# Evicting both banks of turned probabilities with one instruction per engine in place of two, in a one-core attention and MLP kernel

## The reference

```
mask   = q_assign[:, :, :, None] == k_assign[:, :, None, :]
scores = scale * np.matmul(q, k.transpose(0, 1, 3, 2))
scores = np.where(mask, scores, -1000000000.0)
attn   = np.exp(scores - max) / (sum + 1e-09)
out    = np.matmul(attn, v)
```

## Time and profile before

| | us |
|---|---|
| median of 3 runs | 789.22 |
| lowest and highest | 788.41, 789.59 |
| time of the profiled execution | 788.7 |
| its span, first to last instruction | 786.9 |
| attention, first to last turn (L1069) | 24.0 to 300.0 |

### The profile page before, as it was taken

One profiled execution on the slowest core, in us unless ns is written; L12 is line 12 of the kernel. 1 busy time (PEld: TensorE's weight loads), 2 busy tenths in 40 slices (PEclk: granted clock), 3 DMA queues, 4 the chain that ended last, 5 costly groups with the idle time before them and its releaser, 6 DMA issues.

```text
span 786.9 us, 11657 instructions
## 1 busy us (share of the span) xinstructions
PE 738.2 (94%) x4073; PEld 651.2 (83%) x4073; DVE 418.3 (53%) x787; ACT 328.9 (42%) x678; POOL 251.2 (32%) x244
## 2 busy tenths in 40 slices
PE   2899999999999997998999999999999988899998
PEld 1788888888888887997888888888888878898886
DVE  4688788887888888576421141113111158885320
ACT  2677777778777775221111111111101036443311
POOL 5555455556655504002840000000014034641000
PEclk9999999999999999999999999999999999999999
DMA  3223322223343102001310000001013042000011
GB/s 102 70 68 74 92 68 63 63 66 103 109 134 99 43 1 74 35 1 55 108 52 1 0 1 1 1 0 55 1 33 127 1 133 55 28 14 28 27 41 53
DMA packets 20450, 40.93 MB, mean 52 GB/s; under 512 B 2753, under 2 KB 7105, under 8 KB 19905
## 3 DMA queue, kind: packets, MB, share of 16 engines
q1 hardware_dynamic: 17968, 31.62, 14.3%
q0 software_dynamic: 2448, 8.87, 3.4%
HBM read 31.04 MB, written 3.15 MB: 43 GB/s over the span
## 4 chain that ended last, share of the span: by engine, by line
PE 73%; DVE 11%; ACT 8%; issue 6%; POOL 1%; DMA 0%; DVEq 0%; ACTq 0%; SPq 0%; POOLq 0%
PE ps L1162 23%; PE ps L1241 17%; PE ps L1320 9%; PE ps L1306 5%; PE ps L1083 4%; PE ps L1069 4%; PE ps L1057 3%; PE ps L1030 3%; ACT prob L512 2%; PE ps L1058 2%; ACT k L502 2%; DVE row_min L706 2%; ACT pt_h L524 1%; PE ps L1093 1%; ACT q L501 1%
## 5 line engine op out<-in xcount | busy, mean ns | idle before, releaser
L924 DVE SCALAR_TENSOR_TENSOR hid_l<-ps,hid_h 128x512 fp32r<-128x512 f32 x48 | 33.2, 691 | 203.0 <-ACT hid_h L612 203.0
L713 DVE TENSOR_TENSOR pt_l<-ps,pt_h 128x384 fp32r<-128x384 f32 x192 | 102.5, 551 | 47.5 <-ACT pt_h L524 47.2
L612 ACT ACTIVATE hid_h<-ps 128x512 fp32r<-128x512 f32 x48 | 28.7, 598 | 227.0 <-PE ps L1162 227.0
L524 ACT ACTIVATE pt_h<-ps 128x384 fp32r<-128x384 f32 x192 | 84.0, 489 | 48.8 <-PE ps L1069 48.2
L706 DVE TENSOR_REDUCE row_min<-ps 128x1 f32<-128x768 f32 x96 | 90.3, 940 | 6.5 <-PE ps L1058 6.5
L512 ACT ACTIVATE prob<-ps,row_min 128x768 f32<-128x768 f32 x96 | 86.8, 905 | 1.9 <-DVE row_min L706 1.5
L1069 PE MATMUL ps<-cst,prob 128*128 128x128 f32 x576 | 83.4, 282 | 2.9 <-ACT prob L512 2.8
L1057 PE MATMUL ps<-k,q 80*128 80x384 f32 x192 | 74.9, 390 | 3.4 <-ACT k L502 1.5
L1162 PE MATMUL ps<-un_h,w_h 128*128 128x512 f32 x192 | 75.7, 394 | 1.4 <-DVE un_l L918 1.4
L1241 PE MATMUL ps<-w_h,hid_h 128*128 128x512 f32 x192 | 76.0, 396 | 0.0
L1162 PE MATMUL ps<-un_l,w_h 128*128 128x512 f32 x192 | 75.6, 394 | 0.0
(11 more groups left out here) (138 smaller groups left out, 1570.8 us busy)
## 6 DMA issues: line engine op xcount, KB each, us to landing
stage<-in_moe_w_ch SPq DMA_DIRECT2D x16, 256.0 KB, 3.3
w_raw<-in_moe_w_ch SPq DMA_DIRECT2D x16, 256.0 KB, 2.6
raw_qk<-in_q SPq DMA_DIRECT2D x16, 192.0 KB, 3.2
raw_qk<-in_k SPq DMA_DIRECT2D x16, 192.0 KB, 3.4
raw_v<-in_v SPq DMA_DIRECT2D x16, 192.0 KB, 2.5
q<-q SPq DMA_DIRECT2D x16, 192.0 KB, 2.6
k<-k SPq DMA_DIRECT2D x16, 192.0 KB, 2.6
out<-out_s SPq DMA_DIRECT2D x12, 256.0 KB, 2.0
```

What stands on the lines that cost most here:

```text
L524: nc.scalar.activation(pt_h[a][:, R * hf:R * hf + R, (t % R) * P:(t % R + 1) * P], ps[:, 4 + hf, 0:HALF].rearrange("p (j c) -> p j c", j=R ...
L713: nc.vector.tensor_tensor(pt_l[a][part], ps[:, 4 + hf, 0:HALF].rearrange("p (j c) -> p j c", j=R), as_f32(pt_h[a][part]), ALU.subtract).th ...
```

## The change

Both halves are evicted together. TensorE waits once for `low_ready` before the six transposes, and counts `turn_ready` once behind the sixth. `store_high` is one Copy of 768 columns from banks 4 and 5, and `store_low` one subtraction of 768 columns. The counts of the semaphores halve. VectorE's instructions of the mask chain, which stood between two halves of `store_low`, now stand behind the whole; `denominator` is moved in the same way.

```diff
             def store_high(n, t):
-                for hf in range(2):
-                    act.wait_ge(turn_ready, 2 * g + hf + 1)
-                    if t % R == 0 and hf == 0 and not (isinstance(n, int) and n == 0):
-                        act.wait_ge(o_ready, AHEAD + 2 * n + a - 1)
-                    nc.scalar.activation(
-                        pt_h[a][:, R * hf:R * hf + R, (t % R) * P:(t % R + 1) * P],
-                        ps[:, 4 + hf, 0:HALF].rearrange("p (j c) -> p j c", j=R),
-                        ACT.Copy).then_inc(high_ready, 1)
+                act.wait_ge(turn_ready, g + 1)
+                if t % R == 0 and not (isinstance(n, int) and n == 0):
+                    act.wait_ge(o_ready, AHEAD + 2 * n + a - 1)
+                nc.scalar.activation(
+                    pt_h[a][:, :, (t % R) * P:(t % R + 1) * P].rearrange("p (h j) c -> p h j c", h=2),
+                    ps[:, 4:6, 0:HALF].rearrange("p h (j c) -> p h j c", j=R),
+                    ACT.Copy).then_inc(high_ready, 1)
...
-            def store_low(n, t, hf):
+            def store_low(n, t):
                 g, a = 6 * n + t, t // R
-                dve.wait_ge(high_ready, 2 * g + hf + 1)
...
+                dve.wait_ge(high_ready, g + 1)
+                part = (slice(None), slice(None), slice((t % R) * P, (t % R + 1) * P))
+                nc.vector.tensor_tensor(pt_l[a][part].rearrange("p (h j) c -> p h j c", h=2),
+                                        ps[:, 4:6, 0:HALF].rearrange("p h (j c) -> p h j c", j=R),
+                                        as_f32(pt_h[a][part]).rearrange("p (h j) c -> p h j c", h=2),
+                                        ALU.subtract).then_inc(low_ready, 1)
...
-                store_low(m, 1, 0)
+                store_low(m, 1)
                 if prep2:
                     add_dots(n + 2)
-                store_low(m, 1, 1)
                 if prep2:
                     largest_dot(n + 2)
                 minimum(m, 1 - s, 3)
                 if prep2:
                     hits(n + 2)
-                store_low(m, 2, 0)
+                store_low(m, 2)
                 if prep2:
                     weigh_hits(n + 2)
-                store_low(m, 2, 1)
                 if prep2:
                     first_hit(n + 2)
                     masks(n + 2)
...
                 pe.wait_ge(exp_ready, g + 1)
+                if not (isinstance(g, int) and g == 0):
+                    pe.wait_ge(low_ready, g)
                 for hf in range(2):
-                    if not (isinstance(g, int) and g == 0):
-                        pe.wait_ge(low_ready, 2 * g - 1 + hf)
                     for j in range(R):
                         last = nc.tensor.transpose(ps[:, 4 + hf, j * P:(j + 1) * P],
                                                    prob[t % 2][:, R * hf + j, :], ident)
-                    last.then_inc(turn_ready, 1)
+                last.then_inc(turn_ready, 1)
```

More of the change, by code:

```diff
@@ L509, in exponent @@
                 if not (isinstance(g, int) and g < 2):
-                    act.wait_ge(turn_ready, 2 * g - 2)
+                    act.wait_ge(turn_ready, g - 1)
                 col = 6 * s + t
@@ L707, in minimum @@
                                         axis=AX.XY, op=ALU.min).then_inc(min_ready, 1)
-            def store_low(n, t, hf):
+            def store_low(n, t):
                 g, a = 6 * n + t, t // R
-                dve.wait_ge(high_ready, 2 * g + hf + 1)
-                part = (slice(None), slice(R * hf, R * hf + R), slice((t % R) * P, (t % R + 1) * P))
-                nc.vector.tensor_tensor(pt_l[a][part], ps[:, 4 + hf, 0:HALF].rearrange("p (j c) -> p j c", j=R),
-                                        as_f32(pt_h[a][part]), ALU.subtract).then_inc(low_ready, 1)
+                dve.wait_ge(high_ready, g + 1)
[4 more added lines that the diff above has]
+                                        ALU.subtract).then_inc(low_ready, 1)
             def add_dots(n):
@@ L775, in step @@
             def step(n, s, t, more=True):
-                store_low(n, t, 0)
-                store_low(n, t, 1)
+                store_low(n, t)
                 if t < 4:
@@ L794, in head @@
                 step(n, s, 4, more=prep1)
-                store_low(n, 5, 0)
+                store_low(n, 5)
                 denominator(n, s, 0)
-                store_low(n, 5, 1)
                 invert(n, 0)
@@ L807, in head @@
                 minimum(m, 1 - s, 1)
-                store_low(m, 0, 0)
+                store_low(m, 0)
                 denominator(n, s, 1)
-                store_low(m, 0, 1)
                 invert(n, 1)
@@ L1070, in turn @@
                                                    prob[t % 2][:, R * hf + j, :], ident)
-                    last.then_inc(turn_ready, 1)
+                last.then_inc(turn_ready, 1)
             def values(n, s, a, part):
                 if part == 0:
-                    pe.wait_ge(low_ready, 12 * n + 6 * a + 6)
+                    pe.wait_ge(low_ready, 6 * n + 3 * a + 3)
                     pe.wait_ge(v_split, n + 1)
```

## The result

The changed kernel takes 820.65 us (median of 4, 819.88 to 824.62) against 788.82 before: a ratio of 1.0414, with a 95% interval of 1.0392 to 1.0437. The forecast was 803.0 with a range of 798.5 to 808.0. The sign was right and the size was not: of the 32 us lost, the sum had 14.

A forecast was written before the change was run, and what follows sets the result against it. TensorE's work bounds most of a head, a VectorE and ScalarE chain bounds m3; heads 10.2, end 2.0, behind the last turn 0.6 and opening 1.0 make 13.8 us more, forecast 803.0, range 798.5 to 808.0.

The forecast's parts named there:

- heads, loop and mask chain: In the 14 heads with a mask, the mask comes 0.73 us later in each: 10.2 us.
- opening steps: Three first steps that wait in the same way, at the loop's 0.37 us each: about 1.0 us.
- end, to the last turn: Six last steps without a mask, 2.76 us each, 16.56 in place of 14.54: 2.0 us more.
- behind the last turn: VectorE's last low part starts later, with the next stage's subtractions behind it: 0.6 us.
- Low path: From turn to turn through Copy and subtraction of 768 columns: 2.71 to 2.76 us, becoming the loop over TensorE's 2.44.
- the replay: One head stepped through from the turn of m1, Copy starting at 0.85, mask turn at 6.81 us, before 6.08.
- the mask chain: VectorE's work from m1 to the mask turn in m3: the mask comes 0.73 us later.
- its cover: In t5 the loop of 2.76 us fits under the step's 3.01: no cost.
- Faster: Rival: fewer VectorE starts shorten the mask chain of m1 and m2; 2.0 us less, 787.2; chance 0.03.
- Hidden: Rival: late turns of m1 and m2 only eat into TensorE's waits; only the ends cost 3.6, 792.8; chance 0.06.
- Slow forms: Rival: the two-bank Copy and subtraction run at their upper bounds; 811 us; chance 0.08.
- Clock: Rival: idling TensorE falls to half clock in one step a head; 34 us more, 837; chance 0.01.

The follow-up runs named there:

- e2: Changed kernel with GpSimd's `split_v` of a head waiting for that head's mask (`mask_ready`); 807.26 us.
- e10: Kernel before the change with only GpSimd's `split_v` waiting for the mask; 787.46 us, ratio 0.9982.
- e1: Changed kernel without VectorE's `denominator`: the 1e-9 is left out and `invert` reads `row_sum` itself; 815.84 us.
- e4: Control: kernel before the change, with `denominator` left out and `split_v` waiting for the mask; 786.83 us, ratio 0.9977.
- e9: Kernel before plus GpSimd's wait for the mask; TensorE counts `turn_ready` once, so ScalarE's first Copy waits for six transposes; all instructions in halves; 805.67 us.
- e5: Kernel before plus GpSimd's wait for the mask; `turn_ready` counted once, one Copy of 768 columns, subtraction and TensorE's turn wait still in halves; 804.64 us.
- e7: Kernel before plus GpSimd's wait for the mask; only the waits merged (ScalarE for six transposes, turn for both low halves), four instructions in halves; 806.11 us.
- e11: Kernel before plus GpSimd's wait for the mask, VectorE's mask chain one place forward, one k mask eviction moved from ScalarE to VectorE; 781.82 us, ratio 0.9905.

## Why the prediction was wrong

Its sum, term by term, against the traces (14 heads with a mask):

| term | predicted | measured | from |
|---|---|---|---|
| heads, loop and mask chain | 10.2 | 13.7 | 14 x (18.38 - 17.40), e2 |
| `masks` beside GpSimd | 0 | 9.0 | 14 x (4.50 - 3.86), m3 |
| `denominator` beside GpSimd | 0 | 6.2 | 14 x (3.27 - 2.83), m1 |
| opening steps | 1.0 | 2.4 | 16.6 - 14.2 |
| end, to the last turn | 2.0 | 2.4 | 20.0 - 17.6 |
| behind the last turn | 0.6 | 0 | 487.5 in both |
| start of the first turn | 0 | -1.2 | 22.84 against 24.05 |
| sum | 13.8 | 32.5 | spans: 32.3 |

The first two rows set e2, in which GpSimd waits, against the kernel before, in which it does not. Against e10, which has the same wait, the heads' loop and chain are 14 x (18.38 - 17.29) = 15.3, and `masks` is so much less (7.4, since the kernel before already lost 1.5).

**The step that failed** is the sentence on the other engines: "GpSimd, SyncE and their DMAs get no instruction and no wait more; their waits are on steps that come later, and so start later with them". That is true and beside the point. It looked at what GpSimd waits for, and put what VectorE meets beside it at nothing. GpSimd's work on v starts when the values of m2 are through, so it moves with TensorE: 2.80 behind the turn of m2 before, 2.79 now. `masks` stands 2.99 behind that turn before and 3.35 now. Before, `masks` ran from 121.91 to 122.50: it lost 0.17 to GpSimd's first instruction for v (121.72 to 122.23) and was nearly through when the subtraction for v started at 122.32. Now it starts with that subtraction, and its second instruction waits for the end of it.

The other half of the failed step is "VectorE's `denominator` and `invert` stand behind a whole low part now; they are read by `store_x`, which waits for `fold_o`, so no cost". Behind the whole low part `denominator` starts 2.63 or 2.71 us behind the turn of m0, where it was 1.58 or 1.66. GpSimd's first instruction on k stays about where it was behind that turn, 2.31 to 3.36 now and 2.58 to 3.28 before. So a margin of 0.96 to 1.70 us fell to between -0.40 and 0.65, which is why 8 heads pay and 6 do not. The two together are 15.2 of the 18.7 us that the sum was short. e2 takes `masks` out and e1 `denominator`, and e4 shows that the kernel before has only the 0.17 a head of `masks`. The largest of the other misses are m0, 14 x 0.19 = 2.7, and the opening, 1.4.

The Trainium skill, SBUF — State Buffer, section SBUF: two separate sides, states the mechanism: VectorE and GpSimd share a pair of ports as an exclusive lock, taken for a whole instruction by a VectorE instruction in a two-port mode or with two inputs in SBUF (this one only against a GpSimd instruction that reads SBUF), or by a GpSimd one; who starts first has it, the other blocks. For VectorE the traces agree, down to the first come (0.03 us behind GpSimd costs `denominator` 1.25, 0.01 ahead nothing). For GpSimd they show little of a block: its subtraction takes 1.07 to 1.08 when the first mask instruction, 0.26 long, started just ahead of it, and 1.00 to 1.01 in e2. That the ports are the cause is the Trainium skill's account; what the runs show is that the start times decide. `masks` has two inputs in SBUF; the subtraction to `pt_l` has one of its two in PSUM and runs beside GpSimd unhindered (958 ns in the mean, 955 alone). `denominator` has one input, in SBUF; which of these kinds it is, no run shows.

**The loop was right in kind and 0.07 to 0.12 us short.** Low path predicted at 2.71 to 2.76, measured 2.83. Its terms are: Copy behind the turn 0.88, at 126.06 for the turn at 125.18 (0.85 to 0.90 predicted); Copy 812 ns (0.82); subtraction 954 (0.95); the release of the turn 0.15, from the low part's end at 125.03 to 125.18, for which the sum had 0.06, taken from another wait. In m0 the Copy starts at 123.23, 0.99 behind its turn, and m0 was put at no cost and costs 0.19. That Copy, like the one of m3, has a second wait, for `o_ready`. It was late in the kernel before too (0.62 behind the turn in m0 and m3, 0.54 in m1, means of the heads), and the replay took m1's value; whether the `o_ready` wait is the reason was not tried.

The opening was under-counted: its second, third and fourth steps grew from 3.00, 2.56 and 3.62 to 3.53, 3.50 and 4.53, where the sum had 0.37 each. Six transposes take 1.51 to 1.54 us there, in the kernel before only 1.05 and 0.90 from its third turn on; so the merged waits weigh more, at a granted clock that reads full. The 0.6 behind the last turn did not come. Two smaller readings were off: the prediction's own rows have 0.10 to 0.15 from Exp's end to the next turn, not 0.06 (2.39 less 2.29), and its 1.65 us of TensorE waits in a head stands in no row; TensorE is idle 0.81 of the 17.40.

**What held.** Durations of both merged instructions; the mask chain: in e2 m1, m2 and m3 together are 0.75 longer than before (9.54 against 8.79), where 0.73 was forecast. That close a match is in part luck: against e10, with the same wait of GpSimd, they are 0.84 longer. t5 kept its cover (3.02 to 3.04). The stages behind attention took 487.5 us in both. The first turn starts between 22.75 and 24.07 over all these kernels, so its -1.2 is no effect of the change.

**The rivals.** *Faster* fell: m1 and m2 are 2.80 and more in the changed kernel, where it needed 2.44. *Hidden* fell: e2's head is 0.98 longer. *Slow forms* fell: 812 and 954 ns. *Clock* fell: every slice reads full. None of them was two engines that fall in step; the result lies beyond the range because a cause that the traces could have shown, GpSimd's timeline laid beside VectorE's, was not priced. The rule of the Trainium skill that the prediction weighed (Perfetto Trace Analysis, section Optimizing Scalar/DVE Operations: breaking up instructions where these engines aren't saturated but cause bubbles) points the right way here, and e9 sharpens it for ScalarE: it is not the size of the Copy that costs but the grain of its wait. e9 has the small instructions and a coarse wait, and costs as much as e5. For the subtraction the two were not parted.

## What to carry to other kernels

Before merging two instructions that work on two banks, ask what the next engine could do after the first half: a semaphore that now counts once puts a serial path together (turn, Copy, subtraction, turn), and e7 (806.1) costs as much as e2 (807.3) though its instructions are not merged. When a change shifts one engine against another by some tenths of a microsecond, lay GpSimd's timeline beside VectorE's and look for small VectorE instructions in SBUF that now start just behind a GpSimd one; a wait that keeps the two apart, one line as in e2, was worth 13 of the 32 us here. It is no cure for good: GpSimd's work behind it moves as well, and e10 and e11 show new meetings (`denominator` up to 1.14, `hits` up to 0.96 in e11). Look at every head and not at one. Where a step is bound by one engine's serial evictions, as t4 by ScalarE's, give one of them to an idle engine (e11).

## What the runs showed of the hardware

- A `denominator` of 128x3 takes 0.16 us, and up to 1.41 when GpSimd started first; it was held over two GpSimd instructions on end (0.82 and 0.61, from 124.88 to 126.28), until the second had ended.
- The order of two starts decided between 0.16 and 1.41 us: `denominator` took 0.16 when it started 0.01 us ahead of GpSimd, and 1.41 when it started 0.03 us behind.
- A subtraction of 128x768 with one input in PSUM took 958 ns in the mean where it ran wholly beside GpSimd and 955 where it ran alone; `masks` and `hits`, with both inputs in SBUF, took 1.05 in place of 0.25 and up to 0.96 in place of 0.35 (changed kernel, e11).
- ScalarE's two Copies of 384 columns from two banks take 0.87 together and one of 768 takes 0.81: merging them wins 0.06 us of ScalarE a step. VectorE's pair takes 1.01 to 1.02 and the merged one 0.954.
- What a released turn needs after its releaser's end differs: 0.06 behind `masks` and behind e7's low half, 0.13 behind Exp in e9, 0.05 behind Exp in the last steps of e7, 0.15 behind the merged low part.
